# An mLSTM with two feed-forward stages: GpSimd's low parts in halves, two sums made earlier, x sums in two parts

## The reference, cut to what matters

```python
for t in range(S):                     # B, H, S, D = 2, 8, 768, 40
    C = f * C + i * outer(v_t, k_t)    # gated recurrent state per head
    y_t = sigmoid(o_t) * (C @ q_t) / max(|n . q_t|, 1)
x = y as (1536 tokens, 320)
h = x @ w_in                           # layer one: 320 -> 2048
x = (h - tanh(h)) @ w_out              # 2048 -> 320
p = probs / (sum(probs) + 1e-9)        # layer two: 4 experts, 320 -> 1024 -> 320
out = sum over e of p[:, e] * (relu(x @ w1[e]) @ w2[e])
```

## Time and profile before

| what | value |
|---|---|
| median of 3 runs | 573.78 us (573.66 to 574.08) |
| profiled execution, its own time | 573.42 us |
| its span, first to last instruction | 571.6 us |
| PE busy | 563.1 us, 99% |
| DVE, POOL, ACT busy | 341.5, 257.8, 245.8 us |
| bytes moved by DMA | 48.08 MB |

### The profile page before, as it was taken

The page is one execution under the profiler, slowest core; times in us unless marked ns, Lnnn a source line. Parts: engine busy times, 40 slices in busy tenths (PEclk is TensorE's granted clock), DMA queues, the critical chain, the costliest instruction groups (busy, mean ns, idle before and its releaser), DMA issues.

```text
span 571.6 us, 10100 instructions
## 1 busy us (share of the span) xinstructions
PE 563.1 (99%) x3796; PEld 539.9 (94%) x3796; DVE 341.5 (60%) x655; ACT 245.8 (43%) x501; POOL 257.8 (45%) x250
## 2 busy tenths in 40 slices
PE   9999999999999999999999999999999999999997
PEld 8999999999998877799999999999999999999997
DVE  6656556565554577676844764645665654764644
ACT  5785645555534555544333432234422245322221
POOL 4988423333202668776417881037780047820000
PEclk9999999999999999999999999999999999999999
DMA  7987446654225022060002320003220012000201
GB/s 264 355 292 229 155 129 166 172 169 99 63 63 146 9 60 60 2 155 21 1 2 76 95 71 1 0 3 110 69 61 2 1 44 77 1 0 1 71 2 69
DMA packets 46359, 48.08 MB, mean 84 GB/s; under 512 B 21830, under 2 KB 36422, under 8 KB 46310
## 3 DMA queue, kind: packets, MB, share of 16 engines
q1 hardware_dynamic: 46208, 47.39, 27.6%
q10 hardware_dynamic: 102, 0.05, 0.0%
HBM read 41.12 MB, written 4.73 MB: 80 GB/s over the span
## 4 chain that ended last, share of the span: by engine, by line
PE 76%; POOL 10%; DVE 7%; ACT 4%; issue 2%; DVEq 0%; POOLq 0%; ACTq 0%
PE bank L1749 7%; PE bank L1751 7%; PE bank L1750 7%; PE bank L1724 5%; PE bank L1727 5%; PE bank L1725 5%; PE bank L1726 5%; PE bank L1706 4%; PE bank L1707 3%; PE bank L1708 3%; PE bank L1679 3%; PE bank L1678 3%; PE bank L1677 3%; POOL fast_w L835 3%; POOL fast_w L831 3%; PE bank L1473 2%
## 5 line engine op out<-in xcount | busy, mean ns | idle before, releaser
L1396 DVE TENSOR_TENSOR x<-bank,x 128x384 f32<-128x384 f32 x160 | 88.7, 554 | 70.9 <-PE bank L1727 69.4
L1749 PE MATMUL bank<-fast_w,g_tiles 128*128 128x320 f32 x384 | 119.1, 310 | 0.0
L1750 PE MATMUL bank<-fast_w,g_tiles 128*128 128x320 f32 x384 | 118.7, 309 | 0.0
L1751 PE MATMUL bank<-fast_w,g_tiles 128*128 128x320 f32 x384 | 118.6, 309 | 0.0
L1073 ACT ACTIVATE g_tiles<-x 128x384 fp32r<-128x384 f32 x96 | 50.4, 525 | 143.8 <-DVE x L1396 143.4
L1390 DVE SCALAR_TENSOR_TENSOR g_tiles<-x,g_tiles 128x384 fp32r<-128x384 f32 x96 | 68.8, 724 | 17.7 <-ACT g_tiles L1073 14.2
L831 POOL TENSOR_TENSOR fast_w<-fast_raw,fast_w 128x512 fp32r<-128x512 f32 x16 | 21.4, 1336 | 120.4 <-ACT fast_w L1014 120.4
L1750 PEld LDWEIGHTS bank<-fast_w,g_tiles 128*128 128x128 f32 x384 | 72.6, 189 | 0.0
L1749 PEld LDWEIGHTS bank<-fast_w,g_tiles 128*128 128x128 f32 x384 | 72.4, 188 | 0.0
L1751 PEld LDWEIGHTS bank<-fast_w,g_tiles 128*128 128x128 f32 x384 | 72.1, 188 | 0.0
L1343 DVE TENSOR_TENSOR bank<-bank,g_tmp 128x384 f32<-128x384 f32 (+2 forms) x64 | 36.1, 564 | 51.0 <-ACT g_tmp L1028 50.5
(11 more groups left out here) (230 smaller groups left out, 1326.3 us busy)
## 6 DMA issues: line engine op xcount, KB each, us to landing
w_raw<-in_w SPq DMA_DIRECT2D x8, 704.0 KB, 7.2
zb<-z SPq DMA_DIRECT2D x10, 512.0 KB, 4.9
feat<-in_feat SPq DMA_DIRECT2D x10, 512.0 KB, 4.1
fast_raw<-in_w SPq DMA_DIRECT2D x16, 320.0 KB
tok<-in_tok SPq DMA_DIRECT2D x10, 484.0 KB, 4.6
fast_raw<-in_w SPq DMA_DIRECT2D x16, 256.0 KB
fast_raw<-in_w SPq DMA_DIRECT2D x32, 128.0 KB
spare<-xg SPq DMA_DIRECT2D x8, 256.0 KB, 2.7
```

What stands on the lines that cost most here:

```text
L1396: V.tensor_tensor(out, bank_of(u, name)[:, 0:WIDE], other, ALU.add).then_inc(summed, 1)
L1749: mm(out, g_tiles[:, k, 0, c], high_w, start=first, stop=False)
L1750: mm(out, g_tiles[:, k, 0, c], low_w, start=False, stop=False)
L1751: mm(out, g_tiles[:, k, 1, c], high_w, start=False, stop=stop).then_inc(third_done, 1)
```

## The change: what it does

- `low_weights`: the two up instructions of the first four blocks become two of 256 columns each, the down one two of 320 columns; the part of the three sums stays whole and comes last.
- POOL's order for experts 1 to 3: the sums of the fourth piece come ahead of the low parts of the third.
- `add_x` and `add_x_parts` become `add_x_main(h)` (rows that need no spreading) and `add_x_tails(h)`. For half 0 the first is ahead of the sums of piece 0, the second behind them.
- `xa_high` and `xa_low`: the steps in which ACT and DVE make the blocks of half 0 change.
- DVE in units 1 to 31: the sum of C21 (product 4) and `mix(v, 3)` come ahead of the low part of C22.

```diff
@@ -483,8 +483,8 @@
         split_at = {0: -1, 1: -1, 2: 1, 3: 4, 4: 5, 5: 8, 6: 9, 7: 11}
 
 
-        xa_high = {50: (B11,), 51: (B21,), 52: (B22,), 55: (T1, T2), 59: (T3, T4)}
-        xa_low = {53: B11, 54: B21, 55: B22, 56: T1, 58: T2, 60: T3, 61: T4}
+        xa_high = {50: (B11,), 51: (B21,), 52: (B22,), 55: (T1, T2), 56: (T3, T4)}
+        xa_low = {52: (B11, B21), 53: (B22,), 56: (T1, T2), 58: (T3,), 59: (T4,)}
...
@@ -825,47 +825,57 @@
 
                 w, raw = fast_w[:, q % PPU, :], fast_raw[:, q % FAST_RING, :]
                 pool.wait_ge(sums_of_w, 4 * q + 4)
-                for part, (c, n, src) in enumerate(((0, 4 * P, raw[:, 0:RAW_DN].rearrange("p (m c) -> p m c", m=2)),
-                                                    (4 * P, 3 * P, sums_in(q)[:, :, :]))):
-                    pool.wait_ge(high_up, 2 * q + part + 1)
-                    G.tensor_tensor(w[:, F_LOW + c:F_LOW + c + n], src[:, 0, :], w[:, c:c + n].bitcast(F32),
+                src = raw[:, 0:RAW_DN].rearrange("p (m c) -> p m c", m=2)
+                pool.wait_ge(high_up, 2 * q + 1)
+                for half in range(2):
+                    c = slice(half * 2 * P, (half + 1) * 2 * P)
+                    G.tensor_tensor(w[:, F_LOW + c.start:F_LOW + c.stop], src[:, 0, c], w[:, c].bitcast(F32),
                                     ALU.subtract).then_inc(fast_low, 1)
-                    pool.wait_ge(fast_low, 2 * q + part + 1)
-                    tail_ = w[32:64, F_TAIL + c:F_TAIL + c + n]
-                    G.tensor_tensor(tail_, src[32:64, 1, :], tail_.bitcast(F32), ALU.subtract).then_inc(fast_up, 1)
-                    pool.wait_ge(fast_up, 2 * q + part + 1)
-                    if part == 0:
-                        pool.wait_ge(high_down, q + 1)
-                        G.tensor_tensor(w[:, F_DN + 2 * D:F_PIECE], raw[:, RAW_DN:RAW_PIECE],
-                                        w[:, F_DN:F_DN + 2 * D].bitcast(F32), ALU.subtract).then_inc(fast_down, 1)
+                    pool.wait_ge(fast_low, 5 * q + half + 1)
+                tail_ = w[32:64, F_TAIL:F_TAIL + 4 * P]
+                G.tensor_tensor(tail_[:, 0:2 * P], src[32:64, 1, 0:2 * P], tail_[:, 0:2 * P].bitcast(F32),
+                                ALU.subtract).then_inc(fast_low, 1)
+                pool.wait_ge(fast_low, 5 * q + 3)
+                G.tensor_tensor(tail_[:, 2 * P:4 * P], src[32:64, 1, 2 * P:4 * P], tail_[:, 2 * P:4 * P].bitcast(F32),
+                                ALU.subtract).then_inc(fast_up, 1)
+                pool.wait_ge(fast_up, 2 * q + 1)
+                pool.wait_ge(high_down, q + 1)
+                G.tensor_tensor(w[:, F_DN + 2 * D:F_DN + 3 * D], raw[:, RAW_DN:RAW_DN + D],
+                                w[:, F_DN:F_DN + D].bitcast(F32), ALU.subtract).then_inc(fast_low, 1)
+                pool.wait_ge(fast_low, 5 * q + 4)
+                G.tensor_tensor(w[:, F_DN + 3 * D:F_PIECE], raw[:, RAW_DN + D:RAW_PIECE],
+                                w[:, F_DN + D:F_DN + 2 * D].bitcast(F32), ALU.subtract).then_inc(fast_down, 1)
+                c, src = slice(4 * P, BLOCKS * P), sums_in(q)
+                pool.wait_ge(high_up, 2 * q + 2)
+                G.tensor_tensor(w[:, F_LOW + c.start:F_LOW + c.stop], src[:, 0, :], w[:, c].bitcast(F32),
+                                ALU.subtract).then_inc(fast_low, 1)
+                pool.wait_ge(fast_low, 5 * q + 5)
+                tail_ = w[32:64, F_TAIL + c.start:F_TAIL + c.stop]
+                G.tensor_tensor(tail_, src[32:64, 1, :], tail_.bitcast(F32), ALU.subtract).then_inc(fast_up, 1)
+                pool.wait_ge(fast_up, 2 * q + 2)
 
             def x_parts(h):
 
                 return ((T1, plain(h, -1), plain(h, B11)), (T2, plain(h, B22), x_sum(h, T1)),
                         (T3, plain(h, B22), plain(h, -1)), (T4, plain(h, B21), x_sum(h, T2)))
 
-            def add_x():
-
-                pool.wait_ge(x2_main, 6)
-                pool.wait_ge(tails_in, 128)
-                for i, one, two_ in x_parts(0):
-                    after(pool, x_sums, i - T1)
-                    G.tensor_tensor(x_sum(0, i), one, two_, ALU.subtract).then_inc(x_sums, 1)
-
-            def add_x_parts():
-
-
-                pool.wait_ge(x2_main, 8)
-                pool.wait_ge(block_ready, BLOCKS)
-                pool.wait_ge(xt_ready, len(L1_SIZES))
-                for i, one, two_ in x_parts(1):
-                    after(pool, x_main_sums, i - T1)
-                    G.tensor_tensor(x_sum(1, i)[:, 0, :], one[:, 0, :], two_[:, 0, :], ALU.subtract).then_inc(x_main_sums, 1)
-                pool.wait_ge(x_main_sums, 4)
-                pool.wait_ge(tails_in, 256)
-                for i, one, two_ in x_parts(1):
-                    after(pool, x_sums, 4 + i - T1)
-                    G.tensor_tensor(x_sum(1, i)[:, 1, :], one[:, 1, :], two_[:, 1, :], ALU.subtract).then_inc(x_sums, 1)
+            def add_x_main(h):
+
+                pool.wait_ge(x2_main, 6 + 2 * h)
+                if h:
+                    pool.wait_ge(block_ready, BLOCKS)
+                    pool.wait_ge(xt_ready, len(L1_SIZES))
+                for i, one, two_ in x_parts(h):
+                    after(pool, x_main_sums, 4 * h + i - T1)
+                    G.tensor_tensor(x_sum(h, i)[:, 0, :], one[:, 0, :], two_[:, 0, :], ALU.subtract).then_inc(x_main_sums, 1)
+
+            def add_x_tails(h):
+
+                pool.wait_ge(x_main_sums, 4 * h + 4)
+                pool.wait_ge(tails_in, 128 * (h + 1))
+                for i, one, two_ in x_parts(h):
+                    after(pool, x_sums, 4 * h + i - T1)
+                    G.tensor_tensor(x_sum(h, i)[:, 1, :], one[:, 1, :], two_[:, 1, :], ALU.subtract).then_inc(x_sums, 1)
 
...
+            add_x_main(0)
             add_weights(0)
-            add_x()
+            add_x_tails(0)
             for q in range(PPU):
                 low_weights(q)
                 if q + 1 < PPU:
                     add_weights(q + 1)
-            add_x_parts()
+            add_x_main(1)
+            add_x_tails(1)
             for i in (T1, T2, T3, T4):
                 x_block_low(i)
             pool.wait_ge(down_done, L1_STEPS)
@@ -896,8 +908,8 @@
                 low_weights(q)
                 low_weights(q + 1)
                 add_weights(q + 2)
+                add_weights(q + 3)
                 low_weights(q + 2)
-                add_weights(q + 3)
                 low_weights(q + 3)
 
         @block.scalar
@@ -1381,8 +1393,8 @@
                     evac(m // L1_TILES - 1)
                 if m in down_at:
                     high_of_down(down_at[m])
-                if m in xa_low:
-                    x_block_low(0, xa_low[m])
+                for i in xa_low.get(m, ()):
+                    x_block_low(0, i)
 
             def low_tile(u, k, src):
 
@@ -1430,10 +1442,9 @@
                 add_product(u, 5, sum_b, sum_b)
                 if ends:
                     mix(v, 2)
+                    mix(v, 3)
+                add_product(u, 4, sum_c, sum_a)
                 low_tile(u, C22, sum_b)
-                add_product(u, 4, sum_c, sum_a)
-                if ends:
-                    mix(v, 3)
                 dve.wait_ge(summed, 5 * u + SUM_C21)
                 add_product(u, 3, sum_a, sum_a)
                 low_tile(u, C21, sum_c)
```

## The result

| | before | after |
|---|---|---|
| median of six runs | 573.72 us | 568.45 us (567.98 to 569.34) |
| ratio of the two | | 0.990, 95% interval 0.9878 to 0.9923 |
| profiled execution, its own time | 573.42 | 568.09 |
| its span | 571.6 | 566.3 |

The changed kernel is 5.3 us faster; the forecast was 6.5 (567.3, range 566.2 to 569.6).

What follows compares the result with a forecast made beforehand. PE, busy 99% of the span, was taken to bound the kernel, so only its pauses could be won. Gains of 2.4 + 0.85 + 3.25 = 6.5 us gave 566.9, plus 0.36 for the median: 567.3 us, range 566.2 to 569.6.

Steps and rivals of the forecast that it cites:

- the three stretches: Where PE pauses: layer-one tail (3.5 us lost), units 1 to 4 (0.95), units 9, 10 and their likes (3.7).
- Units 0 to 4: Pauses at the starts of units 1 to 4 mostly go, unit 0 left alone: gain 0.85 us, bounds 0.5 and 0.95.
- Units 9, 10 and their likes: Pauses for piece 7's sums and C21's sum vanish; per unit pair 1.24 lost becomes 0.15, 3.25 us in all.
- 0.15 lost in each of units 8, 16 and 24: POOL's halves delay piece 6's sums by 0.78 against 0.79 slack: 0.15 us lost per unit, bounds 0 and 0.6.
- Rival 4: C12's sum, behind C22's low part, comes late for product 6 in 15 units: slower, 575.5 us; chance 0.04.
- The sums of piece 7: Experts: load lands 0.8 after piece 6's add; sums end at 323.3 instead of 329.97, before ACT asks at 327.4.
- The tail: Layer one, `up(53)` to first expert product: 1.05 of 3.5 us lost stays, gain 2.4, bounds 1.0 and 3.1.
- T1 and T2: Four low parts in step 56 against POOL's add of piece 1: PE loses 0.35 us, bounds 0 to 0.7.
- Steps 60 and 61 have no block any more, so 0.5 and 0.8 go: Layer-one tail: with x blocks moved out of these steps, pauses of 0.5 and 0.8 us disappear.
- rival 1: The wait on POOL moves to units 8, 16, 24, PE losing 0.8 us in each: 569.3 us; chance 0.13.
- Rival 2: Pairing x blocks builds pauses as large as those removed; tail gains only 0.7 us: 569.0 us; chance 0.15.
- Rivals 3 and 4: The first: hardly any effect, PE's pauses having another last releaser, 572.8 to 573.8 us, chance 0.04; the second: see Rival 4.

Runs made afterwards that it cites:

- all_three: Changed kernel with sums moved ahead of some low parts in POOL's order, in layer one and in the experts, and T1's low part in step 55: 565.95 us.
- c21_first: Kernel before with one edit, C21's sum and `mix(v, 3)` ahead of C22's low part: 570.91 us.
- whole_pieces: Changed kernel with the halves undone, POOL's low parts being whole instructions again: 567.91 us.
- t1_sooner: Changed kernel with T1's low part in step 55 instead of 56: 567.63 us.
- piece_sums_sooner: Changed kernel where, for pieces 1 and 2 of layer one, POOL makes the down part's low parts behind the next piece's sums: 567.88 us.

## Why the prediction was right, and where it was off

- **PE's pauses bound the kernel, and 8.2 us was the most to be had**: right. The gain of the changed kernel and of all_three is found in the three stretches; the latter wins 3.3 + 0.95 + 3.7, 8.0 us of it, and its median is 7.9 below.
- **DVE is held for whole POOL instructions**: right. Of the x blocks' low parts in the tail of the kernel before, ten are held, by 0.35 to 1.0 us, and each ends 0.41 or 0.42 us after the end of a POOL instruction that it met. In the changed kernel there are five. The halves alone take 3.0 us out of the tail.
- **Units 0 to 4**: 0.85 forecast, 0.84 measured; c21_first alone gives 0.96. That it fits so well is luck: the 0.1 that was to stay in unit 4 is gone, and 0.11 is lost in unit 1 instead. whole_pieces does not have it.
- **Units 9, 10 and their likes**: both pauses went as forecast. What is mis-sized is the term "0.15 lost in each of units 8, 16 and 24": it measured 0.34, so the three groups won 2.69 and not 3.25. The cost of the halves was not the reason: the three more instructions took 0.76 where 0.78 was taken (POOL took 5.04 us instead of 4.28 up to the part of the three sums of piece 5, from 305.93 and from 308.03), and the sums behind them came only 0.5 to 0.65 later by it. The other 0.52 came through C12's sum, ACT and POOL's start. Unit 8 took 10.51 us, outside the 10.2 to 10.4 that was to be seen. Rival 4 named that sum's lateness, but looked only at product 6 of PE and not at the copies that stand behind it in ACT's queue.
- **The sums of piece 7**: POOL waited 1.57 us for their load (0.8 in the prediction), but they ended at 321.47 and ACT's copy began at 324.88, so it cost nothing.
- **The tail**: 2.4 forecast, 1.82 measured, inside the bounds. B22 cost 0.17 where 0.3 was taken, T1 and T2 0.59 where 0.35 was; T3 and T4 cost nothing where 0.05 and 0.35 were. The step that failed is "Steps 60 and 61 have no block any more, so 0.5 and 0.8 go". DVE had no block, but ACT's copy in step 60 waited 1.8 us for POOL's sums of piece 2 and PE lost 0.9. I had followed POOL's cost into the units and not into step 60, and had taken DVE's lateness in step 56 as a price for PE alone. t1_sooner and piece_sums_sooner each remove the pause, by its first and by its last link, and the runs without halves don't have it.
- **Rivals**: rival 1's outcome (the wait moves to unit 8) came at 0.34 us where it named 0.8, and half of it by POOL's late start and not by a dearer piece. Rival 2 (pairing) came in the one pair T1 and T2, at 0.6 and with the follow-up of 0.9. Rivals 3 and 4 did not decide the time.
- **The sum**: the two misses, 0.6 in the tail and 0.56 in the groups, have the same sign and don't cancel; they are the 1.2 us between forecast and result.

## What to carry to other kernels

When an engine runs late, list everything that stands behind the late instruction on every queue that it feeds: PE loses only what exceeds its slack, but ACT and POOL carry the whole delay on, and it can come out five steps later. Cutting POOL's instructions pays where DVE is held behind them (3.0 us here), and costs where POOL's own end is awaited (2.0 us); move the awaited result ahead of the work nobody waits for, and both can be had. Edits that each remove pauses don't add up: measure them by stretches between fixed instructions, alone and together.

## What was not expected of the hardware

- POOL's instructions repeat to about 0.02 us where DVE leaves them alone (0.74 for 256 columns, 0.88 for 320, 1.29 for 512), so that the cost of three more, 0.76 us, is close to the 0.78 worked out from other sizes.
- The hold goes both ways. In the changed kernel T3's second low part takes 0.99 us instead of 0.55 behind POOL's instruction of 215.87, and POOL's own take 1.05 and 1.08 us there instead of 0.73 and 0.88.
- The start of `up(53)` lay between 192.11 and 193.46 us in the fourteen profiled executions, although no edit but those of the x sums works ahead of it. That 1.3 us is a large part of the spread between runs, and the stretches behind it don't contain it.
